# The first two query tiles of a fused attention and feed-forward kernel: another way to their scores and values, two more unsplit units, and a score block moved

## Chip, cores and metric

One core of one Trainium2 chip runs the whole program. The metric is the device time of that core in microseconds, the median of several executions. Five engines matter: TensorE (PE in the profile; PEld is its weight load), VectorE (DVE), ScalarE (ACT), GpSimd (POOL) and SyncE (SP), which issues all transfers.

## What is computed

Attention of 12288 queries over 768 pooled keys, and then two feed-forward layers. All widths are 128 (C), the hidden width F is 2048.

```python
kv_pool = kv.reshape(B, H // r, r, W // r, r, C).mean(axis=(2, 4))     # r = 4: 16 pixels a key
kv_flat = kv_pool.reshape(B, -1, C) @ w_sr                             # 768 x 128
k = v = kv_flat
s = scale * (q @ k.transpose(0, 2, 1))                                 # scale = 1/sqrt(128)
s = s - s.max(-1, keepdims=True)
a = np.exp(s); a /= a.sum(-1, keepdims=True) + 1e-09
x = a @ v
h = x @ w_in1;  g = where(h >= 1, h, where(h <= -1, 0, (h + 1)**2 / 4));  y1 = g @ w_out1
h = y1 @ w_in2; g = h * sigmoid(1.702 * h);                               out = g @ w_out2
```

## The kernel before

**Layout.** Everything lies with channels, keys or hidden columns on the 128 partitions and queries along the free axis. The queries come in 24 tiles of T = 512. A tile needs scores in KC = 6 chunks of 128 keys, a maximum over keys, the exponential, values (six chunks again), a division by the sum, and U = 8 *units* for each layer. A unit is 256 hidden columns: `layer_in` makes 128 x 1024 hidden values in PSUM, ScalarE and VectorE apply the nonlinearity, and `layer_out` adds the unit's part into `ps_y1` or `ps_y2`.

**Split arithmetic.** Precision comes from splitting each operand into an upper (fp32r) and a lower part and running three one-pass matmuls (`three_passes`, L469 to L471: upper by upper, upper by lower, lower by upper). The lower parts of the hidden values are made by GpSimd (`lower`, L380), the upper ones by VectorE (L1043) for layer 1. A *plain* unit does without: `layer_out_plain` (L595) multiplies unsplit fp32 values by the raw weights, as two matmuls, each of them two records in the trace. In the kernel before, the first PLAIN = U = 8 units of layer 1, the whole of tile 0, are plain in their output half.

**Pools and first keys.** Twelve groups of 64 keys arrive by 512 KB transfers (L311). VectorE sums each (`TENSOR_REDUCE`, L882) into `window_sum`. TensorE runs 16 records of matmuls whose result nobody reads while the sums arrive (L704), then projects keys (L476) and values (L482). Keys and the first queries are split, and tiles 0 and 1 are scored in three passes a chunk.

**Tile 0** has its own path. VectorE takes the maxima from PSUM, folds them to 32 rows, and spreads them with an identity pattern into `spread_hi` and `spread_lo`, which twelve matmuls with `minus_ones` subtract in PSUM (L523). ScalarE takes exponentials out of PSUM (L767). Values are six plain matmuls `v_sb` by `s_sb` (L554), with channels on the partitions. In parallel VectorE adds the keys (`add_first_keys`), matmuls sum over partitions (L532), VectorE inverts, a matmul spreads the inverse (L538), ScalarE copies it, and VectorE multiplies into `x_hi`, `x_sb` and `x_lo` (`normalise_first`).

**Later tiles.** The scores are copied to SBUF (by ScalarE for tiles 1 to 3, `evacuate`), VectorE folds the maxima (`maximum`, `fold_maximum`), SP stores the 512 maxima to DRAM and loads them back over all partitions (`spread_max`), VectorE subtracts (`shift`, L993), ScalarE exponentiates (L773), VectorE adds over keys (`add_keys`, L999) and inverts (`invert`, which holds the small `TENSOR_TENSOR` of L1015), and SP spreads the inverse in the same way. `normalise` and `x_lower` follow.

**Order.** Each engine has its list written by hand. From iteration 4 on it is a loop body: the scores of tile `it`, the values of tile `it-2`, then eight steps k. Step (it, k) runs layer 1's unit n = 8*it + k - 18 and layer 2's unit n = 8*it + k - 29, with the output halves two and one steps behind. The three iterations before this are written out: steps (2, 2) to (2, 7), then the values of tile 1 and the scores of tiles 2 and 3 together, then steps (3, 0) to (3, 7). GpSimd has its own list, in which the splits of the weights `w_in1`, `w_in2`, `w_out2` and `w_out1` (numbers 0, 2, 3, 1) lie between the waits, and `w_out1`'s lower halves are made in place of the raw weights only after the plain units have used them.

## Time and profile before

| | us |
|---|---|
| median of 3 runs (1302.08 to 1303.64) | 1302.35 |
| profiled execution, its own time | 1302.89 |
| its span in the trace | 1301.1 |
| PE busy | 1272.7 (98%) |
| POOL busy | 1140.8 (88%) |
| ACT busy, DVE busy | 1006.5, 1002.9 (77% each) |

The profiled time is 1.8 us more than the span. Most of the span is the loop, in which each of the 24 tiles takes the same time; the first tenth holds the hand-written start. A row of the timeline gives start, duration, engine, line, operation, output and inputs, the number of instructions merged, and in brackets the idle time before them and what ended it. The records of neighbouring matmuls overlap, so the pitch from one start to the next is what a matmul costs.

### The profile page before, as it was taken

What the parts mean: (1) busy time and instruction counts of PE and PEld (TensorE: products, weight loads), DVE (VectorE), ACT (ScalarE), POOL (GpSimd) and SP (SyncE); (2) the same over time, 40 slices, a digit from 0 to 9 for tenths busy, and PEclk for the clock granted to TensorE, in tenths of its full rate; (3) what the DMA queues carried; (4) which work ended last, traced back from release to release, by engine and by line L of the source; (5) the groups of instructions that cost most, each with busy time, mean ns of one, the idle gap of its engine ahead of it and who ended that gap; (6) DMA issues with size and microseconds to landing.
All of it is one profiled execution on the core that took longest, in us unless ns stands there. A gap on an engine that the chain in (4) does not pass through costs nothing.

```text
span 1301.1 us, 17012 instructions
## 1 busy us (share of the span) xinstructions
PE 1272.7 (98%) x5492; PEld 1027.3 (79%) x5492; DVE 1002.9 (77%) x1151; ACT 1006.5 (77%) x1069; POOL 1140.8 (88%) x476
## 2 busy tenths in 40 slices
PE   6989999999999999999999999999999999999998
PEld 4456888888888888888888888888888888888876
DVE  7877878779778787797797877967978878776443
ACT  3677787888877878888778788878787888797666
POOL 3538999999999999999999999999999999979780
PEclk9999999999999999999999999999999999999999
DMA  9010001000000010010000000100001000000000
GB/s 345 28 33 9 17 17 33 17 18 33 16 16 16 16 32 16 16 32 16 16 16 16 32 16 16 32 16 16 16 16 32 16 17 25 9 17 17 1 9 17
DMA packets 18258, 35.72 MB, mean 27 GB/s; under 512 B 3248, under 2 KB 3376, under 8 KB 17968
## 3 DMA queue, kind: packets, MB, share of 16 engines
q1 hardware_dynamic: 18224, 35.30, 8.3%
q8 instruction: 18, 0.29, 0.1%
q14 instruction: 16, 0.13, 0.0%
HBM read 28.90 MB, written 6.39 MB: 27 GB/s over the span
## 4 chain that ended last, share of the span: by engine, by line
PE 89%; POOL 5%; issue 3%; DVE 1%; ACT 1%; DMA 1%; POOLq 0%; SPq 0%; ACTq 0%; DVEq 0%
PE ps_ring L469 17%; PE ps_ring L471 16%; PE ps_ring L470 16%; PE ps_y L469 13%; PE ps_y L470 12%; PE ps_y L471 12%; POOL g_lo L380 4%; PE ps_y L595 1%; PE ps_y L554 1%; DMA kv_sb<-in_kv_t 1%; PE ps_k L704 0%; POOL pt_lo L380 0%; DVE g L1052 0%; POOLq L48 0%; DVE s_third L993 0%
## 5 line engine op out<-in xcount | busy, mean ns | idle before, releaser
L380 POOL TENSOR_TENSOR g_lo<-g,g_hi 128x1024 fp32r<-128x1024 f32 x365 | 930.2, 2577 | 89.7 <-DVE g L1052 80.0
L1043 DVE SCALAR_TENSOR_TENSOR g_hi<-g,ps_ring 128x1024 fp32r<-128x1024 f32 x184 | 223.9, 1217 | 145.0 <-ACT g L815 142.9
L796 ACT ACTIVATE g<-ps_ring 128x1024 f32<-128x1024 f32 x192 | 197.2, 1027 | 171.5 <-PE ps_ring L471 171.3
L469 PE MATMUL ps_y<-g_hi,w_hi 128*128 128x512 f32 x752 | 296.7, 394 | 8.1 <-POOL g_lo L380 6.9
L470 PE MATMUL ps_y<-g_lo,w_hi 128*128 128x512 f32 x752 | 293.2, 390 | 0.0
L471 PE MATMUL ps_y<-g_hi,w_lo 128*128 128x512 f32 x752 | 293.0, 390 | 0.0
L1052 DVE SCALAR_TENSOR_TENSOR g<-g,ps_ring 128x1024 f32<-128x1024 f32 x192 | 232.9, 1213 | 5.0 <-ACT g L815 5.0
L815 ACT ACTIVATE g<-g 128x1024 f32<-128x1024 f32 x192 | 204.3, 1064 | 5.4
L808 ACT ACTIVATE g<-ps_ring 128x1024 f32<-128x1024 f32 x192 | 197.7, 1030 | 8.6 <-PE ps_y L595 6.4
L798 ACT ACTIVATE g_hi<-ps_ring 128x1024 fp32r<-128x1024 f32 x192 | 195.8, 1020 | 6.2 <-PE ps_y L471 6.2
L469 PEld LDWEIGHTS ps_y<-g_hi,w_hi 128*128 128x128 f32 x752 | 141.1, 188 | 46.8 <-POOL g_lo L380 10.6
L471 PEld LDWEIGHTS ps_y<-g_hi,w_lo 128*128 128x128 f32 x752 | 141.3, 188 | 29.9
L470 PEld LDWEIGHTS ps_y<-g_lo,w_hi 128*128 128x128 f32 x752 | 141.4, 188 | 28.1
L469 PE MATMUL ps_ring<-x_hi,w_hi 128*128 128x512 f32 x382 | 151.7, 397 | 0.7 <-ACT s_sb L733 0.7
L380 POOL TENSOR_TENSOR pt_lo<-s_sb,pt_hi 128x1024 fp32r<-128x1024 f32 x60 | 151.4, 2552 | 0.0
L469 PE MATMUL ps_ring<-y_hi,w_hi 128*128 128x512 f32 x384 | 150.1, 391 | 0.0
L470 PE MATMUL ps_ring<-y_lo,w_hi 128*128 128x512 f32 x384 | 149.9, 390 | 0.0
L471 PE MATMUL ps_ring<-y_hi,w_lo 128*128 128x512 f32 x384 | 149.6, 390 | 0.0
L471 PE MATMUL ps_ring<-x_hi,w_lo 128*128 128x512 f32 x382 | 148.7, 389 | 0.0
L470 PE MATMUL ps_ring<-x_lo,w_hi 128*128 128x512 f32 x382 | 148.7, 389 | 0.0
L993 DVE TENSOR_TENSOR s_sb<-s_sb,key_max 128x1024 f32<-128x1024 f32 x66 | 126.5, 1919 | 0.0
L896 DVE COPY s_sb<-ps_ring 128x512 f32<-128x512 f32 x120 | 80.9, 688 | 52.7 <-PE ps_ring L471 52.7
(127 smaller groups left out, 1680.4 us busy)
## 6 DMA issues: line engine op xcount, KB each, us to landing
kv_sb<-in_kv_t SPq DMA_DIRECT2D x12, 512.0 KB, 9.0
q_sb<-in_q_t SPq DMA_DIRECT2D x24, 256.0 KB, 3.7
out_t<-y_sb SPq DMA_DIRECT2D x24, 256.0 KB, 3.6
key_max<-max_row SPq DMA_DIRECT2D x23, 256.0 KB, 3.4
inv_sum<-inv_row SPq DMA_DIRECT2D x23, 256.0 KB, 3.3
w_raw<-in_moe_w_in SPq DMA_DIRECT2D x2, 1024.0 KB, 17.4
max_row<-max_turned SPq DMA_DIRECT2D x23, 2.0 KB, 1.3
inv_row<-inv_turned SPq DMA_DIRECT2D x23, 2.0 KB, 1.3
```

What stands on the lines that cost most here:

```text
L380: return nc.gpsimd.tensor_tensor(dst, src, upper.bitcast(F32), ALU.subtract)
L469: nc.tensor.matmul(dst, l_hi, r_hi, start=start, stop=False)
L470: nc.tensor.matmul(dst, l_hi, r_lo, start=False, stop=False)
L471: return nc.tensor.matmul(dst, l_lo, r_hi, start=False, stop=stop)
L796: nc.scalar.activation(g2[:, slot, :], ps_h2(it, k), ACT.Gelu_apprx_sigmoid).then_inc(g2_done, 1)
L798: nc.scalar.activation(g2_hi[:, slot, :], ps_h2(it, k), ACT.Gelu_apprx_sigmoid).then_inc(g2_hi_done, 1)
L808: nc.scalar.activation(g, ps_h1(it, k), ACT.Relu, bias=0.5, scale=0.5).then_inc(relu_done, 1)
L815: nc.scalar.activation(g, g, ACT.Square).then_inc(square_done, 1)
L896: nc.vector.tensor_copy(s_sb[:, half, c, :], ps_s(it, c)).then_inc(s_evac, 1)
L993: nc.vector.tensor_tensor(pair, pair, key_max[:, :].unsqueeze(1).to_broadcast([P, 2, T]), ALU.subtract).then_inc(shifted, 1)
L1043: nc.vector.scalar_tensor_tensor(out=g1_hi[:, uu % 2, :], in0=g1[:, uu % 2, :], scalar=1.0, in1=ps_h1(it, k), op0=ALU.min, op1=ALU.max).th ...
L1052: nc.vector.scalar_tensor_tensor(out=g, in0=g, scalar=1.0, in1=ps_h1(it, k), op0=ALU.min, op1=ALU.max).then_inc(g1_done, 1)
```

## The change

1. **Tile 0 and 1 are scored by projected queries.** `w_sr` is transposed by a matmul, the queries are projected by it (`project_q`), and the score chunk is one plain matmul of `window_sum` by the projected queries (`whole_scores`). It needs neither projected keys nor split queries. The 16 unread matmuls are gone.
2. **GpSimd sums four of the twelve groups** (0, 3, 6, 9) by a tree of four additions; VectorE sums eight and takes the maxima of the score chunks between them.
3. **One spread of the maxima** with upper and lower part on different partitions: six matmuls in place of twelve.
4. **Tile 0's values with queries on the partitions**: for each key chunk four plain matmuls with 128 queries as weights and 129 moving columns, the last of them ones, so that the sums stand beside the values. ScalarE copies them out, and four matmuls by a diagonal of the inverses turn and scale them (`first_inputs`).
5. **Tile 1's score chunks 1 to 5 move** to after tile 0's values, between the first steps of layer 1.
6. **PLAIN = U + 2**: units 0 and 1 of tile 1 are plain too. `w_out1`'s lower parts are made in three pieces: units 2 and 3, units 4 to 7, and units 0 and 1 late.
7. **Tile 3 is scored after steps (3, 0) and (3, 1)**, not together with tile 2. ScalarE's, VectorE's and GpSimd's lists follow.

```diff
-        PLAIN = U
+        PLAIN = U + 2
+            def wait_sums(eng, group):
+                by_pool = sum(1 for g in POOL_GROUPS if g <= group)
+                at_least(eng, summed, group + 1 - by_pool)
+                at_least(eng, pool_summed, by_pool)
...
# GpSimd
+            def sum_windows(turn, g):
+                keys = slice(g * GK, (g + 1) * GK)
+                pool.wait_ge(kv_loaded[g], 16)
+                for level, width in enumerate((8, 4, 2)):
+                    if level:
+                        pool.wait_ge(windows_halved, turn * 3 + level)
+                    nc.gpsimd.tensor_tensor(kv_sb[:, keys, 0:width], kv_sb[:, keys, 0:width],
+                                            kv_sb[:, keys, width:2 * width], ALU.add).then_inc(windows_halved, 1)
+                pool.wait_ge(windows_halved, turn * 3 + 3)
+                nc.gpsimd.tensor_tensor(window_sum[:, keys].unsqueeze(2), kv_sb[:, keys, 0:1], kv_sb[:, keys, 1:2],
+                                        ALU.add).then_inc(pool_summed, 1)
...
-            q_lower(0, q_lo[:, :], q_sb[:, 0, :], q_hi[:, :])
-            pool.wait_ge(k_copied, 1)
-            pool.wait_ge(k_hi_done, 1)
...
+            for turn, g in enumerate(POOL_GROUPS):
+                sum_windows(turn, g)
             w_upper(0, 0)
+            pool.wait_ge(max_masked, 1)
             w_lower(0, 0)
-            pool.wait_ge(max_masked, 2)
             w_upper(0, 1)
             w_lower(0, 1)
-            pool.wait_ge(x_lo_done, 1)
+            pool.wait_ge(k_copied, 2)
+            pool.wait_ge(k_hi_done, 2)
+            pool.wait_ge(inverse_masked, 1)
+            lower(k_lo[:, :], k_sb[:, :], k_hi[:, :]).then_inc(k_lo_done, 1)
...
-            pool.wait_ge(g1_used, PLAIN - U // 2)
-            w_lower(1, 0)
+            pool.wait_ge(g1_used, U // 2)
+            w_out1_lower(PLAIN - U, U // 2 - 1)
+            pool.wait_ge(g1_used, U)
+            w_out1_lower(U // 2, U - 1)
             for k in range(U):
                 step(3, k)
-                if k == 4:
+                if k == 6:
                     pool.wait_ge(g1_used, PLAIN)
-                    w_lower(1, 1)
+                    w_out1_lower(0, PLAIN - U - 1)
...
# TensorE
+            def whole_scores(t, c):
+                if c == 0:
+                    pe.wait_ge(q_copied, t + 1)
+                if t == 0:
+                    wait_sums(pe, 2 * c + 1)
+                nc.tensor.matmul(ps_s(t, c), window_sum[:, c * P:(c + 1) * P], q_proj[:, t, :], start=True,
+                                 stop=True).then_inc(scores_ready, 1)
...
+                for b in range(QUADS):
+                    last = nc.tensor.matmul(ps_o_turned(b), s_sb[:, 0, c, b * P:(b + 1) * P], v_sb[:, c, 0:C + 1],
+                                            start=(c == 0 and b % 2 == 0), stop=(c == KC - 1), skip_group_check=True)
...
+                for b in range(QUADS):
+                    last = nc.tensor.matmul(ps_y1[:, b * P:(b + 1) * P], o_t[:, b, :], inv_diag[:, b, :], start=True,
+                                            stop=True)
...
+            turn_projection()
+            project_q(0)
+            for c in range(FIRST_CHUNKS):
+                whole_scores(0, c)
+            project_v(0)
             project_k(0)
...
+            whole_scores(0, 4)
+            project_q(1)
+            whole_scores(0, 5)
+            whole_scores(1, 0)
+            project_v(1)
+            project_k(1)
+            subtract_maximum()
             for c in range(KC):
-                score_chunk(1, c)
...
-            sum_first_keys()
-            value_chunk(0, 4)
-            spread_inverse()
-            value_chunk(0, 5)
-            for k in range(U):
+                first_values(c)
+            whole_scores(1, 1)
+            first_inputs()
+            whole_scores(1, 2)
+            step(2, 0, 2)
+            whole_scores(1, 3)
+            whole_scores(1, 4)
+            pe.wait_ge(s_early, 3)
+            step(2, 0, 3)
+            whole_scores(1, 5)
+            pe.wait_ge(s_early, 5)
+            for k in range(4, U):
                 step(2, 0, k)
-            values_then_scores(1, 2, 3)
-            for k in range(U):
+            values_then_scores(1, 2)
+            for k in range(2):
+                step(3, 1, k)
+            for c in range(KC):
+                score_chunk(3, c)
+            step(3, 1, 2)
+            pe.wait_ge(s_early, 3 * KC)
+            for k in range(3, U):
                 step(3, 1, k)
             iterations(pe, iteration)
...
# ScalarE, from the first step on
             step(2, 0, 2)
+            evacuate_chunk(1, 1, 3)
+            evacuate_chunk(1, 1, 4)
             step(2, 0, 3)
+            evacuate_chunk(1, 1, 5)
             step(2, 0, 4)
+            step(2, 0, 5)
             exponential(1, 1, 0)
-            step(2, 0, 5)
             exponential(1, 1, 1)
+            step(2, 0, 6)
             exponential(1, 1, 2)
-            step(2, 0, 6)
             step(2, 0, 7)
             evacuate(2, 0)
-            evacuate(3, 1)
+            step(3, 1, 0)
+            step(3, 1, 1)
+            for c in range(4):
+                evacuate_chunk(3, 1, c)
             x_upper(1, 1)
-            for k in range(U):
+            evacuate_chunk(3, 1, 4)
+            evacuate_chunk(3, 1, 5)
+            for k in range(2, U):
                 step(3, 1, k)
...
# VectorE, after tile 0
             maximum(1, 1, 2)
-            normalise_first()
             fold_maximum(1)
-            unit_full(2, 2)
-            unit_full(2, 3)
+            unit_full(2, 4)
+            unit_full(2, 5)
             shift(1, 1, 0)
-            unit_full(2, 4)
             shift(1, 1, 1)
             shift(1, 1, 2)
-            unit_full(2, 5)
+            unit_full(2, 6)
+            unit_full(2, 7)
             for p in range(PAIRS):
                 add_keys(1, 1, p)
-            unit_full(2, 6)
             invert(1)
-            unit_full(2, 7)
             for p in range(PAIRS):
                 maximum(2, 0, p)
             fold_maximum(2)
+            unit_full(3, 0)
+            unit_full(3, 1)
             normalise(1)
             x_lower(1, 1)
-            for p in range(PAIRS):
-                maximum(3, 1, p)
+            maximum(3, 1, 0)
+            shift(2, 0, 0)
+            maximum(3, 1, 1)
+            shift(2, 0, 1)
+            maximum(3, 1, 2)
...
-                if k < U - 1:
+                if 1 < k < U - 1:
                     unit_full(3, k)
...
                 if k == 2:
                     shift(2, 0, 2)
+                if k == 3:
+                    fold_maximum(3)
```

## Rows read from the trace of the kernel before

**Rows 1.** Busy time by stretch: us, then busy us and instructions of each engine

```profile
88.10:123.00 34.90, 28.62 (x105) 20.47 (x105) 30.70 (x33) 26.48 (x27) 27.74 (x12) 0.95 0.08 23
135.00:1301.10 1166.10, 1160.54 (x5093) 952.98 (x5091) 898.70 (x1017) 925.55 (x973) 1066.91 (x431) 1.00 0.06 19
```

**Rows 2.** The key groups' transfers: issues (ns, first to last start), and time to landing

```profile
L311 SPq DMA_DIRECT2D kv_sb<-in_kv_t x12: 417/442/655, 1.2 to 7.6; - x12
...
DMA to landing us min/median/max: 3.9/9.0/12.9
```

**Rows 3.** Timeline of tile 0: DVE, ACT, PE, and ACT at the first unit

```profile
9.01 12.71 DVE L882 TENSOR_REDUCE window_sum<-kv_sb 128x64 f32<-128x1024 f32 x10 [1.49 <-DMA kv_sb<-in_kv_t]
...
31.73 2.85 ACT L767 ACTIVATE s_sb<-ps_ring 128x1024 f32<-128x1024 f32 x3 [1.22 <-PE ps_ring L523]
...
32.90 3.67 PE L554 MATMUL ps_y<-s_sb,v_sb 128*128 128x512 f32 x8 [0.30 <-ACT s_sb L767]
...
43.74 1.03 ACT L808 ACTIVATE g<-ps_ring 128x1024 f32<-128x1024 f32 x1 [1.92 <-PE ps_ring L589]
```

**Rows 4.** Timeline of plain matmuls before 19 us: PE, then its weight loads

```profile
11.63 2.47 PE L704 MATMUL ps_k<-window_sum,w_k 128*128 128x256 f32 x5 [11.63 <-DVE window_sum L882]
...
17.62 0.86 PEld L482 LDWEIGHTS ps_v<-w_v,window_sum 128*128 128x128 f32 x7 [0.24 <-issue]
```

**Rows 5.** Groups by form, 0 to 60 us: GpSimd's subtractions (busy us, mean ns)

```profile
L380 POOL TENSOR_TENSOR w_lo<-w_raw,w_hi 128x1024 fp32r<-128x1024 f32 x5 | 11.9, 2385 | 0.2
...
L380 POOL TENSOR_TENSOR k_lo<-k_sb,k_hi 128x256 fp32r<-128x256 f32 x2 | 1.4, 730 | 9.8 <-ACT k_sb L733 9.8
```

**Rows 6.** Timeline of PE: plain output halves of two steps that follow each other

```profile
50.44 1.88 PE L595 MATMUL ps_y<-g,w_raw 128*128 128x512 f32 x4
...
53.54 1.88 PE L595 MATMUL ps_y<-g,w_raw 128*128 128x512 f32 x4
```

**Rows 7.** Timeline of ACT: tile 2's score chunks copied out

```profile
66.14 1.30 ACT L733 ACTIVATE s_third<-ps_ring 128x512 f32<-128x512 f32 x2 [0.38 <-PE ps_ring L471]
```

**Rows 8.** Groups by form, 40 to 110 us, DVE

```profile
L1052 DVE SCALAR_TENSOR_TENSOR g<-g,ps_ring 128x1024 f32<-128x1024 f32 x12 | 14.5, 1206 | 5.0 <-ACT g L815 5.0
...
L993 DVE TENSOR_TENSOR s_third<-s_third,key_max 128x1024 f32<-128x1024 f32 x3 | 3.6, 1214 | 0.0
```

**Rows 9.** Timeline of DVE: tile 2's last maximum and the end of its fold

```profile
69.13 1.25 DVE L919 TRANSPOSE_TENSOR_REDUCE part_max<-s_third 128x32 f32<-128x1024 f32 x1 [0.41 <-ACT s_third L733]
...
71.63 0.20 DVE L936 STREAM_TRANSPOSE max_turned<-row_max 32x32 f32<-32x32 f32 x1
```

**Rows 10.** The page's DMA issues: count, KB each, us to landing

```profile
key_max<-max_row SPq DMA_DIRECT2D x23, 256.0 KB, 3.4
...
max_row<-max_turned SPq DMA_DIRECT2D x23, 2.0 KB, 1.3
```

**Rows 11.** Timeline of POOL and DVE where both read SBUF

```profile
46.23 4.71 POOL L380 TENSOR_TENSOR w_lo<-w_raw,w_hi 128x1024 fp32r<-128x1024 f32 x2
...
49.55 2.48 DVE L993 TENSOR_TENSOR s_sb<-s_sb,key_max 128x1024 f32<-128x1024 f32 x1
...
102.20 7.13 POOL L380 TENSOR_TENSOR g_lo<-g,g_hi 128x1024 fp32r<-128x1024 f32 x3
...
107.44 2.97 DVE L993 TENSOR_TENSOR s_sb<-s_sb,key_max 128x1024 f32<-128x1024 f32 x1
```

**Rows 12.** PE's longest idle time after the first unit, and a stretch behind it

```profile
92.64 0.47 PE L469 MATMUL ps_y<-g_hi,w_hi 128*128 128x512 f32 x1 [4.38 <-POOL g_lo L380]
...
94.00:95.00 1.00, 1.00 (x4) 0.81 (x3) 0.00 (x0) 0.98 (x2) 1.00 (x1) 0.50 0.02 8
```

**Rows 13.** Timeline of ACT, DVE and PE at the junction with the loop

```profile
97.25 1.03 ACT L796 ACTIVATE g<-ps_ring 128x1024 f32<-128x1024 f32 x1 [1.24 <-PE ps_ring L471]
...
110.33 1.21 DVE L1043 SCALAR_TENSOR_TENSOR g_hi<-g,ps_ring 128x1024 fp32r<-128x1024 f32 x1
...
132.98 0.50 PE L469 MATMUL ps_y<-g_hi,w_hi 128*128 128x512 f32 x1 [0.59 <-POOL g_lo L380]
```

More of the change, by code:

```diff
@@ L394, in w_lower, with w_out1_lower @@
                 lower(w_lo[:, cols], w_raw[:, cols], w_hi[:, cols]).then_inc(w_lo_done[m], 1)
+            def w_out1_lower(first, last):
+                cols = slice(WF + first * 2 * P, WF + (last + 1) * 2 * P)
+                pool.wait_ge(w_hi_done[1], WP)
+                lower(w_lo[:, cols], w_raw[:, cols], w_hi[:, cols]).then_inc(w_lo_done[1], 1)
             def step(it, k):
@@ L510, in score_chunk @@
                 upper, lower = q_hi, q_lo
-                if is_number(t, 1):
-                    upper, lower = q1_hi, q1_lo
                 if is_number(t, 2):
@@ L518, in subtract_maximum @@
             def subtract_maximum():
-                pe.wait_ge(ones_ready, 2)
-                for part, spread in enumerate((spread_hi, spread_lo)):
-                    pe.wait_ge(max_masked, part + 1)
-                    for c in range(KC):
-                        last = nc.tensor.matmul(ps_s(0, c), minus_ones[:, :], spread[:, :], start=False,
-                                                stop=(part == 1), skip_group_check=True)
-                        if part == 1 and c % 2 == 1:
-                            last.then_inc(max_subtracted, 1)
@@ L528, in sum_first_keys @@
-            def sum_first_keys():
-                pe.wait_ge(s_early, KC)
-                pe.wait_ge(keys_added, 5)
-                for j in range(QUADS):
-                    last = nc.tensor.matmul(ps_y2[:, j:j + 1], key_sums[:, 4, j * P:(j + 1) * P], ones[:, 0:1],
-                                            start=True, stop=True)
-                last.then_inc(first_summed, 1)
-            def spread_inverse():
+                pe.wait_ge(ones_ready, 1)
+                pe.wait_ge(max_masked, 1)
@@ L537, in spread_inverse, with first_inputs @@
+            def first_inputs():
+                pe.wait_ge(o_copied, 2)
                 pe.wait_ge(inverse_masked, 1)
-                nc.tensor.matmul(ps_y2[:, :], ones[:, :], key_sums[:, 0, :], start=True,
-                                 stop=True).then_inc(sums_spread, 1)
+                for b in range(QUADS):
+                    last = nc.tensor.matmul(ps_y1[:, b * P:(b + 1) * P], o_t[:, b, :], inv_diag[:, b, :], start=True,
+                                            stop=True)
+                last.then_inc(x_turned, 1)
@@ L553, in value_chunk @@
                         pe.wait_ge(exp_done, t * PAIRS + (c // 2 + 1))
-                    nc.tensor.matmul(ps_o(t), v_sb[:, c, :], s_keys(t, t % 2, c), start=(c == 0),
+                    nc.tensor.matmul(ps_o(t), v_sb[:, c, 0:C], s_keys(t, t % 2, c), start=(c == 0),
                                      stop=(c == KC - 1)).then_inc(pv_done, 1)
@@ L799, in step @@
                                          ACT.Gelu_apprx_sigmoid).then_inc(g2_hi_done, 1)
+                if k == 3 and is_iteration(it, 3):
+                    y1_upper(it, 1 - half)
                 exists, tt, uu, n = unit(it, k, FIRST1)
@@ L808, in step @@
                     nc.scalar.activation(g, ps_h1(it, k), ACT.Relu, bias=0.5, scale=0.5).then_inc(relu_done, 1)
-                if k == 3 and is_tile(it - 3):
-                    act.wait_ge(g1_used, (it - 3) * U + U)
-                    at_least(act, h2_ready, (it - 4) * U)
-                    copy(y1_hi[:, 1 - half, :], ps_y1[:, :]).then_inc(y1_hi_done, 1)
+                if k == 3 and is_tile(it - 3) and not is_iteration(it, 3):
+                    y1_upper(it, 1 - half)
                 if exists:
```

352 lines of the change are left out of this document (182 added, 170 removed).

## The prediction, made before the changed kernel was run

> **What bounds the kernel now.** I read the engines' busy time by stretch first, and the reader should see in it where time can be won at all. From 135 us on TensorE is busy for 1160.5 of 1166.1 us, while no other engine is [rows 1]. The change leaves that part alone, so all it can do is to let this saturated part begin earlier or later. Between 88 and 123 us TensorE is busy for 28.6 of 34.9 us only [rows 1]: there other engines set the pace. The question is therefore by how much the junction moves at which TensorE waits for the last time, 132.98 us [rows 13]. Then I read the timelines of all engines from 0 to 135 us and followed back what released what. The order of each engine is written by hand, so I lay the changed lists out against each other with durations from this trace. Times below are positions from the span's start.
>
> **Tile 0, first part.** The last kv transfer is issued at 7.6 and lands 12.9 later, at 20.5 [rows 2]. VectorE's ten sums from 9.01 take 1.27 each and so end at 21.7 [rows 3]. Four sums moved to GpSimd do not bring this forward, because the transfer sets it; they free VectorE for maxima. GpSimd's tree adds 512, 256, 128 and 64 elements. Subtractions of 1024 and 256 elements took 2.385 and 0.730 [rows 5], so 2.16 ns an element and 0.18 fixed: 960 elements and four instructions give 2.8, with waits between them 3.2. The short strided runs have no row: the lower bound is 2.8, the upper 4.8, double fixed and element cost for the three small levels. I take 3.2. Groups land about 1.27 apart, so group 9 is there at 17.9 and summed at 21.1, just behind VectorE's pace. Score chunk 4, the projection of tile 1's queries and chunk 5 follow, plain matmuls of 512 columns. A plain one costs 0.86, half of the 1.73 for two that is worked out below from [rows 6]. That gives 23.7. Maximum 0.7, fold and spread 2.3, six subtracting matmuls, of which the first pair is out after 0.7: exponentials from 27.55, against 31.73 [rows 3]. The gain is 4.2.
>
> **Tile 0, second part.** Values start 1.17 behind the first exponential [rows 3], at 28.7. They are 24 matmuls of two records. Seven weight loads of such 128-column records took 0.86 with the last one's 0.19 in it, so 0.11 a record and 0.22 a matmul [rows 4]; sum 5.3, end 34.0. In the old form six chunks at 0.86 make 5.2, so nothing is won there; what goes is the four waits for sums, inverse, its spread and its copy. Small VectorE work on the sums and the diagonal takes 1.2, four turning matmuls 0.9 plus a start, splitting 0.7, the first unit 1.4: its result is out at 38.6. ScalarE took it at 43.74 before [rows 3]. The gain stands at 5.1.
>
> **Tile 1, where it is given back.** Three whole score chunks behind the first unit cost 3 x 0.86 = 2.6 of TensorE, and ScalarE has four more copies to do between the first activations. The unit pace was one step in 3.10 [rows 6]; now activation, square and VectorE's 1.2 [rows 8] of unit 0 and 1 wait behind those copies. VectorE reaches tile 1's last maximum at 46.0 and ends its fold at 48.4 (maximum 1.25 and fold 1.45 after it [rows 9], less overlap). Maxima go through DRAM: 1.3 and 3.4 [rows 10], so the first shift is at 53.1. Then, in ScalarE's new order, two exponentials of tile 1 stand ahead of unit 4: shift 1.2, shift 1.2, exponential 1.0, unit 4's two activations 2.0, exponential 1.0, unit 5's 2.0. That ends at 61.5. TensorE's values of tile 1 end at 61.2 and tile 2's scores follow at ScalarE's pace, 1.30 for two copies after 0.38 of waiting [rows 7], so 5.5 for six chunks with the start: 66.7. Two steps of 3.1 bring TensorE to 73.0. VectorE meanwhile does unit 5, three key sums, the inversion 2.5, three maxima, the fold and unit 6: 61.5 + 1.2 + 3.5 + 2.5 + 3.5 + 1.4 + 1.2, so 74.7 with the gaps. Tile 3's scores wait for this (1.5 idle). x_lo of tile 1 is ready 4.7 later at 79.3, and two steps and a unit (3.1 + 3.1 + 1.4) put the end of unit 10's input at 86.9. In the old trace that point is 92.64 - 4.38 = 88.3 [rows 12]. Of 5.1 won, 1.4 is left.
>
> **The wait behind it.** Before, TensorE idles 4.38 for GpSimd's split of the first split unit, and the following matmuls run at granted clock 0.50, 1.2 GHz [rows 12]. Now units 8 and 9 are plain. Each costs more: a plain step is 3.10, of which six input passes at 0.227 are 1.36, so its output half takes 1.73 against 1.36 split, twice 0.37. What TensorE waits for next is y1's lower part (same bank `ps_y1`). Here a lock decides. A shift that alone takes 1.21 [rows 8] took 2.48 at 49.55, and the subtraction on GpSimd ended at 50.94, 1.39 later; at 107.44 it took 2.97, with GpSimd busy until 109.33 [rows 11]. So VectorE's two-input subtraction in SBUF waits until GpSimd's running instruction ends. In the new lists `w_out1`'s four-unit piece starts on GpSimd when plain unit 7 is done, 6.25 after x_lo, and takes 2.4; tile 2's last shift asks 6.9 after x_lo. It loses 1.75 and ends at 89.0; y1_lo follows at 89.7. Plain unit 8 ends at 91.4, its follower's activations at 93.5, then a table load 1.3, and the first layer 2 activation starts at 94.8, against 97.25 [rows 13]: gain 2.4.
>
> **To the junction.** Units 10 and 11 pass ScalarE and VectorE at the same pace as before, so VectorE ends tile 2's sums with the 2.4. Behind them the old trace lost 1.9 to the lock (107.44 + 2.97 against 1.21). In my layout GpSimd has two fewer hidden subtractions behind it, its subtraction ends at 105.9 and unit 12 comes at 107.0, against 110.33 [rows 13], gain 3.3; if the small addition of 1e-9 in `invert` just misses a gap on GpSimd, all comes 0.9 later, gain 2.4. From there the pattern repeats the old one, since the last `w_out1` piece (1.3) fits into GpSimd's room. VectorE copies tile 4's scores, TensorE waits on them as before, and the junction moves by the same 2.4 to 3.3. I take 2.8.
>
> **The sum.** Span 1301.1 - 2.8 = 1298.3; with the 1.8 outside it, 1300.1 against the profiled 1302.89. That execution lies 0.5 above the median 1302.35, so I forecast 1302.35 - 2.8 = 1299.6.
>
> **Rivals.** (A) *Gains end in slack, no change.* GpSimd's trees at their upper bound delay chunk 4 by 1.6, another loss of the lock costs 0.9 to 1.8, and each moves the chain whole; together the gain is between 2.6 and none: 1299.8 to 1302.4, say 1301.0. For it: the chain has six hand-overs, each placed to a few tenths. (B) *The cold array, slower.* Without the 16 unread records TensorE does little before 20 us. In rows 4 five records of 256 columns in two passes took 2.47, so 0.43 a record, while the later records of 128 columns took 0.11, a quarter for half the columns: the array ran at 1.2 GHz first and at 2.4 GHz later. If it is still at 1.2 GHz until the values are through, chunk 4, the projection, chunk 5 (2.6) and the values (5.3) double: 7.9 against 2.8 won, 1307.4. It decides from 2.8 us of full-speed matmul work on the path that runs at the low clock: chunk 4, the projection and chunk 5 alone (2.6) just take the gain away. Against it: with chunks that cost 1.7 at 1.2 GHz, TensorE is nearly always busy from about 13 us on, as it was before from 11.63, and there the records at 17.62 were the short ones [rows 4]. (C) *More gain.* The last shift of tile 2 gets in ahead of GpSimd (0.65 decides), 1.75 more: 1297.8. (D) *The clock falls again.* TensorE idles 2.8 ahead of plain unit 8, where 4.38 was followed by the low clock [rows 12]; plain unit 8 then costs 1.7 more: 1301.3, within A's time.
>
> The Trainium skill, in "TensorE: Matmul & The Clock Gate", section "Part 1: The HAM clock gate", says that the throttled clock is the default state and activity releases it; that speaks for B, and no row shows how much activity the new start would need.
>
> **Chances.** My forecast with C: 0.50 (C 0.12 of it). A with D: 0.40. B 0.10. A measurement of this kernel tells about 0.2%, 2.6 us, from no change, and the forecast of 2.8 sits on that border, so faster by more is 0.50, within 0.2% is 0.41, and slower by more, B's upper half, is 0.09. The likeliest case's own range is 1297.8 to 1300.7. The whole range leaves out B and the best end of C: 1297.0 to 1303.0.
>
> **What the new profile would show.** First activation of a unit near 38.7 on ScalarE; exponentials of tile 0 near 27.6; weight loads of the turned values 0.11 apart; plain unit 8 near 89.7 behind y_lo; no stretch at clock 0.50 around 94; first layer 2 activation near 94.8; TensorE's last wait near 130.2. I am wrong if the first TensorE records near 20 are still 0.85 apart, if GpSimd's sum of group 9 ends after 22, or if the distance between old and new already differs by more than a microsecond at unit 10's input (86.9 against 88.3).

## The result, and the profile after

The changed kernel takes 1305.7 us (median of 11 runs, 1302.98 to 1308.87). The kernel before, run beside it, takes 1302.95 (11 runs, 1302.08 to 1303.83). The ratio is 1.0022 with a 95% interval from 1.0013 to 1.003, so the change costs 2.75 us and does not win the forecast 2.8. The time lies outside the predicted range, on the other side. The profiled execution took 1305.87, its span is 1304.1. Of the runs of the kernel before that stand beside the experiments, one took 4013.32 us and enters no number below.

The busy times of the changed kernel's page (first part), and the two stretches that answer to [rows 1]:

```profile
PE 1275.8 (98%) x5494; PEld 1023.8 (79%) x5494; DVE 989.8 (76%) x1138; ACT 1006.3 (77%) x1070; POOL 1143.8 (88%) x491
```

```profile
88.10:123.00 34.90, 30.27 (x103) 19.15 (x101) 30.51 (x35) 28.14 (x29) 20.36 (x9) 0.95 0.07 23
135.00:1304.10 1169.10, 1163.06 (x5107) 955.41 (x5105) 901.50 (x1020) 928.45 (x977) 1069.94 (x432) 1.00 0.06 19
```

The loop is as saturated as before. All that the change does happens ahead of the junction, and the junction came later. Its wait, to be set beside the last line of [rows 13], in the timeline of TensorE:

```profile
137.01 0.50 PE L502 MATMUL ps_y<-g_hi,w_hi 128*128 128x512 f32 x1 [0.55 <-POOL g_lo L408]
```

That is 4.03 later than before, while the span is only 3.0 longer: the loop gives 1.0 back, of which more below. The same points that the prediction gave, as it had them, before, and after:

| point | predicted | before | after | after less predicted |
|---|---|---|---|---|
| exponentials of tile 0 start (ACT) | 27.55 | 31.73 | 30.49 | 2.9 |
| first activation of unit 0 (ACT) | 38.6 | 43.74 | 42.21 | 3.6 |
| tile 1's folded maximum stored (SP) | 48.4 | 44.27 | 51.69 | 3.3 |
| first shift of tile 1 (DVE) | 53.1 | 49.55 | 57.46 | 4.4 |
| unit 8's input starts (PE) | 79.3 | 80.10 | 84.50 | 5.2 |
| plain unit 8 (before: split unit 8) | 89.7 | 92.64 | 95.20 | 5.5 |
| first activation of layer 2 (ACT) | 94.8 | 97.25 | 102.17 | 7.4 |
| upper part of unit 12 (DVE) | 107.0 | 110.33 | 114.36 | 7.4 |
| junction (PE) | 130.2 | 132.98 | 137.01 | 6.8 |

The error is made in three places: 2.9 ahead of the exponentials, 2.3 between there and unit 8's input, 1.9 between plain unit 8 and layer 2. The first place, in the timeline of TensorE:

```profile
9.99 2.07 PE L524 MATMUL ps_ring<-q_proj,window_sum 128*128 128x512 f32 x2 [0.69 <-ACT q_proj L801]
...
13.20 3.58 PE L524 MATMUL ps_ring<-q_proj,window_sum 128*128 128x512 f32 x4 [1.13 <-POOL window_sum L404]
...
18.69 1.15 PE L524 MATMUL ps_ring<-q_proj,window_sum 128*128 128x512 f32 x2 [1.91 <-DVE window_sum L977]
19.65 1.89 PE L532 MATMUL ps_two<-wsr_sb,window_sum 128*128 128x128 f32 x8
21.34 1.89 PE L538 MATMUL ps_two<-window_sum,wsr_sb 128*128 128x512 f32 x2
23.05 1.04 PE L524 MATMUL ps_ring<-q_proj,window_sum 128*128 128x512 f32 x2
```

and the same microseconds as stretches (the last three columns are the granted clock, the share of the DMA engines, and GB/s):

```profile
20.00:21.00 1.00, 1.00 (x7) 1.00 (x6) 1.00 (x2) 0.00 (x0) 0.66 (x2) 0.50 1.06 438
21.00:22.00 1.00, 1.00 (x4) 0.67 (x4) 1.00 (x2) 0.42 (x1) 0.00 (x0) 0.50 1.00 418
22.00:23.00 1.00, 1.00 (x2) 0.33 (x1) 0.82 (x1) 0.18 (x1) 0.00 (x0) 0.50 0.95 322
```

There are two slow times here. The first chunk takes 2.07, twice the 1.02 to 1.04 of the same two records later, so TensorE starts at 1.2 GHz; within chunks 1 and 2 it gets faster, and chunk 3 costs 0.96 from its start to the next, at 2.4 GHz. Ahead of chunk 3 TensorE had waited 1.91 for a sum; behind chunk 3 the granted clock falls to 0.50, 1.2 GHz, for some 3.5 us. The two projections of keys and values take 1.89 each, and chunk 4 starts at 23.05 and not at 21.1. GpSimd is not the cause; its last tree, group 9, is through at 20.74:

```profile
17.84 2.53 POOL L401 TENSOR_TENSOR kv_sb<-kv_sb 128x512 f32<-128x512 f32 x3 [0.94 <-DMA kv_sb<-in_kv_t]
20.45 0.29 POOL L404 TENSOR_TENSOR window_sum<-kv_sb 128x64 f32<-128x64 f32 x1
```

Behind the exponentials the price list holds. 48 records of the turned values take 5.60 (predicted 5.3), ScalarE has the first unit's result 11.7 after its first exponential (predicted 11.1):

```profile
31.66 5.60 PE L587 MATMUL ps_two<-v_sb,s_sb 128*128 128x129 f32 x48 [0.27 <-ACT s_sb L850]
```

```profile
30.49 2.86 ACT L850 ACTIVATE s_sb<-ps_ring 128x1024 f32<-128x1024 f32 x3 [1.16 <-PE ps_ring L572]
...
42.21 1.02 ACT L898 ACTIVATE g<-ps_ring 128x1024 f32<-128x1024 f32 x1 [1.04 <-PE ps_ring L647]
```

The maxima of tile 1 then go through DRAM. The second of these issues waits until the first has landed, so their distance is the first's time: 2.31, where it was 1.34 before. Timelines of the DMA queue's issues and of VectorE:

```profile
51.69 0.34 SPq L343 DMA_DIRECT2D max_row<-max_turned  x1
54.00 0.34 SPq L346 DMA_DIRECT2D key_max<-max_row  x1
```

```profile
57.46 1.23 DVE L1060 TENSOR_TENSOR s_sb<-s_sb,key_max 128x1024 f32<-128x1024 f32 x1 [1.66 <-DMA key_max<-max_row]
```

The third place is the wait ahead of plain unit 8. VectorE's last shift of tile 2 waits for GpSimd's piece of `w_out1`, as forecast, and `y_lo` stands behind it. VectorE, GpSimd and TensorE, in three timelines, and the clock of the stretch:

```profile
91.27 3.27 DVE L1060 TENSOR_TENSOR s_third<-s_third,key_max 128x1024 f32<-128x1024 f32 x1
94.47 0.68 DVE L968 TENSOR_TENSOR y_lo<-ps_y,y_hi 128x512 fp32r<-128x512 f32 x1
```

```profile
91.08 2.38 POOL L408 TENSOR_TENSOR w_lo<-w_raw,w_hi 128x1024 fp32r<-128x1024 f32 x1 [16.92 <-PE ps_y L653]
```

```profile
95.20 3.44 PE L653 MATMUL ps_y<-g,w_raw 128*128 128x512 f32 x4 [2.81 <-DVE y_lo L968]
```

```profile
96.00:97.00 1.00, 1.00 (x2) 0.34 (x1) 0.90 (x5) 0.48 (x1) 0.00 (x0) 0.50 0.00 0
```

The shift takes 3.27 for the 1.21 of [rows 8]; it ends 1.08 after the subtraction whose end it waited for, as in [rows 11]. The idle time is 2.81 (forecast 2.8), and what I had put at the end of the list of rivals follows: the clock falls, and four records take 3.44 in place of 1.88 [rows 6].

### The profile page after: what moved, and what is told of

It reads as the page before. It is cut to its first block, busy times and chain, and to the rows that moved or that the text cites. A ratio compares the mean times of both kernels' runs of the same rounds, so it can differ in the third digit from the quotient of the medians.

```text
span 1304.1 us, 17033 instructions
## 1 busy us (share of the span) xinstructions
PE 1275.8 (98%) x5494; PEld 1023.8 (79%) x5494; DVE 989.8 (76%) x1138; ACT 1006.3 (77%) x1070; POOL 1143.8 (88%) x491
## 3 DMA queue, kind: packets, MB, share of 16 engines
HBM read 28.90 MB, written 6.39 MB: 27 GB/s over the span
## 4 chain that ended last, share of the span: by engine, by line
PE 87%; POOL 5%; issue 3%; DVE 2%; ACT 1%; DMA 1%; POOLq 0%; SPq 0%; ACTq 0%; DVEq 0%
PE ps_ring L502 16%; PE ps_ring L503 16%; PE ps_ring L504 16%; PE ps_y L502 12%; PE ps_y L503 12%; PE ps_y L504 12%; POOL g_lo L408 4%; DMA kv_sb<-in_kv_t 1%; PE ps_y L653 1%; PE ps_ring L524 0%; PE ps_two L587 0%; DVE s_third L1060 0%; POOL pt_lo L408 0%; DVE part_max L1000 0%; ACT g L898 0%
```

## The experiments

Three questions: is the low clock at 20 us and at 96 us the cause of the loss; what else lies on the path; and which parts of the change pay. The kernels were timed in three groups (e1 to e4, e5 to e8, e9 to e12), each group on one chip beside the kernel before (medians 1302.89, 1302.91 and 1303.19). None leaves out any of the computation. The stations are the exponentials of tile 0, the first shift of tile 1, the junction, and the first store of maxima in the loop (before 143.73, after 147.75).

| kernel | median us | ratio to before (95%) | exponentials | shift | junction | store in the loop |
|---|---|---|---|---|---|---|
| before | 1302.95 | | 31.73 | 49.55 | 132.98 | 143.73 |
| after | 1305.70 | 1.0022 (1.0013 to 1.003) | 30.49 | 57.46 | 137.01 | 147.75 |
| e1_unread | 1304.21 | 1.0009 (1.0 to 1.0018) | 28.24 | 55.58 | 135.21 | 145.98 |
| e2_y1_first | 1304.89 | 1.0013 (1.0004 to 1.0022) | 30.26 | 57.16 | 134.34 | 145.14 |
| e3_both | 1301.97 | 0.9994 (0.9985 to 1.0003) | 28.14 | 55.40 | 132.57 | 143.34 |
| e4_old_no_unread | 1303.74 | 1.0006 (0.9996 to 1.0015) | 32.80 | 50.63 | 134.60 | 145.39 |
| e5_load_first | 1301.43 | 0.9987 (0.9978 to 0.9996) | 28.25 | 55.03 | 132.20 | 142.96 |
| e6_plain8 | 1304.33 | 1.0011 (1.0002 to 1.002) | 28.23 | 55.60 | 135.08 | 145.85 |
| e7_sums_dve | 1301.33 | 0.9987 (0.9978 to 0.9996) | 28.90 | 55.00 | 132.16 | 142.91 |
| e8_unit4_first | 1303.55 | 1.0003 (0.9994 to 1.0012) | 28.14 | 56.45 | 134.29 | 145.06 |
| e9_fill | 1306.02 | 1.0026 (1.0015 to 1.0037) | 30.29 | 57.51 | 135.64 | 146.41 |
| e10_fill_unread | 1303.43 | 1.0005 (0.9996 to 1.0014) | 28.37 | 55.85 | 134.64 | 145.38 |
| e11_three | 1301.18 | 0.9991 (0.9982 to 1.0) | 29.27 | 55.26 | 132.39 | 143.14 |
| e12_plain12 | 1303.48 | 1.0004 (0.9995 to 1.0013) | 29.35 | 55.25 | 133.27 | 145.24 |

### e1: unread matmuls in the new start

```diff
+            def unread(cols):
+                nc.tensor.matmul(ps_s(0, KC - 1)[:, 0:cols], wsr_t[:, :], q_sb[:, 0, 0:cols], start=True, stop=True)
             for c in range(FIRST_CHUNKS):
                 whole_scores(0, c)
+                if c == 0:
+                    unread(256)
+                if c == 2:
+                    unread(512)
```

> The changed kernel with two unread matmuls put back into TensorE's idle time before chunk 3 (256 and 512 columns). Theory 1 (TensorE at 1.2 GHz from 19.5 to 23 us is what delays the start): those records run at 2.4 GHz, chunk 5 ends near 24.3 in place of 26.3, tile 0's exponentials start near 28.5 in place of 30.5, and the time falls by 2 us to about 1303.7, with less scatter from run to run. Rival (the start is delayed by the hand-overs between engines, and the clock only fills waits): less than 0.5 us.

Two matmuls are added, and the junction comes 1.8 earlier. TensorE's timeline, to be read beside the first fence of after above: chunk 3 starts 0.59 earlier, and the two projections take 1.05 and 1.02 in place of 1.89 each. The 0.59 comes by way of VectorE, which takes the maximum of chunk 2 ahead of the sum that chunk 3 waits for: it starts on it at 16.23, and at 16.82 in the changed kernel, where TensorE's chunks before it were slower.

```profile
18.10 1.13 PE L524 MATMUL ps_ring<-q_proj,window_sum 128*128 128x512 f32 x2 [1.05 <-DVE window_sum L984]
19.07 1.05 PE L532 MATMUL ps_two<-wsr_sb,window_sum 128*128 128x128 f32 x8
19.96 1.02 PE L538 MATMUL ps_two<-window_sum,wsr_sb 128*128 128x512 f32 x2
20.92 1.10 PE L524 MATMUL ps_ring<-q_proj,window_sum 128*128 128x512 f32 x2
```

The exponentials move by 2.25, the shift by 1.88, the junction by 1.80; the median by 1.5, and the runs draw together (1302.77 to 1304.66). The low clock of the start, early and behind chunk 3 together, is worth this much. The second low stretch is still there, behind an idle time of 2.82, and the kernel is still slower than before: the start alone does not explain the loss.

### e2 and e3: `y1_lo` ahead of tile 2's last shift

```diff
                 if k == 3:
...
                     lower(y1_lo[:, 0, :], ps_y1[:, :], y1_hi[:, 0, :]).then_inc(y1_lo_done, 1)
+                    shift(2, 0, 2)
                 unit_upper(3, k)
                 if 1 < k < U - 1:
                     unit_full(3, k)
-                if k == 2:
-                    shift(2, 0, 2)
```

> The changed kernel with VectorE's y1_lo ahead of tile 2's last shift. Theory 1 (that shift waits 2.1 us for GpSimd, TensorE idles 2.8 us behind it and then runs at 1.2 GHz for three more): TensorE's idle time ahead of plain unit 8 falls below 0.6 us, no stretch at clock 0.50 follows, and layer 2's first activation comes 4 us earlier, at 98; the time falls by 3 to 4 us, to about 1302.2. Rival (the shift, not y1_lo, is what the chain needs: the exponentials of tile 2 and unit 10's activation stand behind it): the idle time goes, but the activation comes less than 1.5 us earlier and the time falls by less than 1.5.

> Both edits. Theory 1: the gains add, 5 to 6 us below the changed kernel, about 1300, which is 2 to 3 us below the kernel before and what was forecast. Rival: within 1 us of the better of the two.

In e2 TensorE goes on to plain unit 8 at once, at full clock, and waits 1.43 one step later:

```profile
92.10 1.98 PE L653 MATMUL ps_y<-g,w_raw 128*128 128x512 f32 x4
95.51 0.47 PE L502 MATMUL ps_ring<-y_hi,w_hi 128*128 128x512 f32 x1 [1.43 <-DVE g L1119]
```

The junction comes 2.67 earlier; the median only 0.8, below what I expected. The runs scatter from 1302.78 to 1305.73; why the median does not follow the trace is not shown. With both edits (e3) the junction comes 4.44 earlier, which is 1.80 and 2.67 together, and at 132.57 it is just ahead of the old one. The runs lie between 1301.51 and 1302.43. So the low clock of the start, and the wait with the low clock behind it, together account for 3.7 us of the median; what is left of the change gains 0.9 against the kernel before, within what can be told, and not the forecast 2.8.

### e4: the kernel before without its unread matmuls

```diff
-            for g in range(4, FIRST_GROUPS):
-                pe.wait_ge(summed, g)
-                for _ in range(2):
-                    nc.tensor.matmul(ps_k[:, 3, 0:4 * GK], w_k[:, :], window_sum[:, 0:4 * GK], start=True, stop=True)
```

> The kernel before without its 16 unread matmuls. Theory 1: its first records near 16.7 us run at 1.2 GHz and it loses 2 to 4 us, to about 1305.5, with more scatter. Rival (the old start has slack in its transfers and sums): under 0.7 us.

The exponentials come 1.07 later and the junction 1.62; the median is 0.8 above that of before, less than expected and not separable. The timeline shows where: the first projections run at the low clock, and the scores from the fourth record on do not.

```profile
16.26 2.04 PE L476 MATMUL ps_k<-window_sum,w_k 128*128 128x512 f32 x2 [16.26 <-DVE window_sum L878]
18.10 1.91 PE L482 MATMUL ps_v<-w_v,window_sum 128*128 128x128 f32 x8
20.38 0.77 PE L469 MATMUL ps_ring<-q_hi,k_hi 128*128 128x512 f32 x1 [0.37 <-POOL k_lo L380]
```

Before, the two took 1.04 and 1.05 from 16.74 on. In the traces the old start is therefore 1.62 better at the junction for its 16 matmuls; in the median the price is not shown.

### e5, e7, e11: the way of the maxima, and GpSimd's sums

Each is e3 with an edit. In e5 SP issues the load of tile 4's queries ahead of `spread_max(1)`:

```diff
             load_q(3)
-            spread_max(1)
             load_q(4)
+            spread_max(1)
```

> Both edits (the two unread matmuls, y1_lo first), and the load of query tile 4 issued ahead of the store of tile 1's maxima. Theory 1 (the 2 KB store takes 2.3 to 2.6 us in place of 1.3 because no transfer has run for 15 us or more): the store lands after 1.4 us, tile 1's first shift comes 1.1 us earlier than 55.40, and the junction with the loop moves with it, to 131.5. Rival (the store is slow for another reason, or the shift waits anyway): the shift stays within 0.3 us of 55.40.

The store still takes 2.38 (49.47 to 51.85), so the theory that an idle queue makes it slow has fallen. The median is 0.5 below that of e3, and the interval against the kernel before now leaves out 1.

In e7 VectorE makes all twelve sums again (groups 0 and 3 ahead of the first maximum):

```diff
-    POOL_GROUPS = (0, 3, 6, 9)
+    POOL_GROUPS = ()
...
             first_chunk_maximum(1)
-            first_chunk_maximum(2)
+            sum_windows(6)
             sum_windows(7)
+            first_chunk_maximum(2)
             sum_windows(8)
+            sum_windows(9)
             first_chunk_maximum(3)
```

> Both edits, with all twelve groups summed by VectorE. Theory 1 (the transfers set the sums' pace, and the maxima between them must fit beside): the last chunk's maximum comes after the sums and two maxima are pushed back, 1.0 to 1.5 us on tile 0's exponentials (28.14), same at the junction. Rival (GpSimd's tree of group 9 is the later one and VectorE alone is quicker): exponentials earlier than 28.1.

The exponentials start 0.76 later than in e3, and yet the first shift comes 0.40 earlier, because the store of the maxima takes 1.47 and not 2.60:

```profile
50.11 0.34 SPq L343 DMA_DIRECT2D max_row<-max_turned  x1
51.58 0.34 SPq L346 DMA_DIRECT2D key_max<-max_row  x1
```

So the lead that GpSimd's trees give is real, and in these two traces more than all of it is lost in the store; they bring the time nothing. What goes with a long store is shown in the last section; whether the trees would pay beside a short one was not tried. e11 has both edits, these two diffs on top of e3:

> The unread matmuls at the start, y1_lo first, tile 4's load first, all sums on VectorE. Theory 1 (each of the last two gave 0.4 us at the junction through the maxima's way over DRAM, by different parts of it): 142.5 for the loop's first store in place of 142.9, 1301.0 us. Rival (they give the same 0.4): 142.9, 1301.4.

Its median, 1301.18, is the lowest of the study, but not to be told from 1301.33 and 1301.43: the two gains do not add. The store takes 1.69 there. Any of the three can be kept: they lie 1.5 to 2.0 us below the kernel before by the medians, 1.2 to 1.7 by the ratios.

### e6 and e12: how many plain units

e6 is e3 with two plain units fewer and without the last `w_out1` piece, e12 is e11 with two more:

```diff
-        PLAIN = U + 2
+        PLAIN = U
...
-                if k == 6:
-                    pool.wait_ge(g1_used, PLAIN)
-                    w_out1_lower(0, PLAIN - U - 1)
...
```

```diff
-        PLAIN = U + 2
+        PLAIN = U + 4
...
-            pool.wait_ge(g1_used, U // 2)
-            w_out1_lower(PLAIN - U, U // 2 - 1)
...
-                if k == 6:
+                if k == 7:
                     pool.wait_ge(g1_used, PLAIN)
                     w_out1_lower(0, PLAIN - U - 1)
...
```

TensorE's waits for the pieces follow in both.

> Both edits, with units 0 and 1 of tile 1 split again (PLAIN = 8). Theory 1 (the two unsplit units pay by taking GpSimd's subtractions off the path, more than their 0.73 us on TensorE): TensorE waits for unit 8's lower part, 2 us or more, and the junction comes 1 to 3 us later than 132.57. Rival (with y1_lo early, GpSimd is no longer on the path there): within 0.7 us of 132.57.

> The same, with four unsplit units in tile 1 in place of two. Theory 1 (between 90 us and the junction the chain runs over VectorE and GpSimd, and each unsplit unit takes an upper part of 1.2 and a lower part of 2.4 off them for 0.37 on TensorE): the loop's first store 1 to 2.5 us earlier, near 141. Rival (the chain runs through tile 3's shifts, which the units do not touch, and the last piece of the weights now comes late): no gain, or a new wait at unit 16.

In e6 the old wait for GpSimd is back, with the low clock behind it:

```profile
95.07 0.77 PE L499 MATMUL ps_y<-g_hi,w_hi 128*128 128x512 f32 x1 [4.55 <-POOL g_lo L408]
```

The store in the loop is 2.5 later than in e3, and the median 2.4 higher. This part of the change is worth what the whole was forecast to win. In e12 the work up to 102 us is as in e11, and then TensorE waits 2.88 for a lower part at the junction, where e11 waits 0.58:

```profile
133.27 0.50 PE L500 MATMUL ps_y<-g_hi,w_hi 128*128 128x512 f32 x1 [2.88 <-POOL g_lo L408]
...
134.76 0.61 PE L500 MATMUL ps_ring<-y_hi,w_hi 128*128 128x512 f32 x1
135.17 0.63 PE L501 MATMUL ps_ring<-y_lo,w_hi 128*128 128x512 f32 x1
```

1.5 us after that wait the records go from 0.40 to 0.63 for three to four microseconds. The store in the loop comes 2.1 later than in e11. The median is 2.3 higher: two more plain units cost time.

### e8: unit 4 ahead of tile 1's exponentials

```diff
-            exponential(1, 1, 0)
-            exponential(1, 1, 1)
             step(2, 0, 6)
+            exponential(1, 1, 0)
+            exponential(1, 1, 1)
             exponential(1, 1, 2)
```

VectorE's list follows: `unit_full(2, 6)` ahead of the three shifts.

> Both edits, with unit 4 of tile 0 ahead of tile 1's shifts and exponentials on VectorE and ScalarE. Theory 1 (ScalarE idles for 4 us until the maxima are back while unit 4 lies ready, and then its 2.0 us stand in the chain): unit 5's square, tile 2's scores and all behind them come 1.0 to 2.0 us earlier, the junction near 131. Rival (the chain runs through tile 1's exponentials and values, not through the units): less than 0.4 us.

The store in the loop comes 1.7 later than in e3, against what I expected. TensorE now waits 2.73 for the exponentials, the clock falls, and the values of tile 1 take 7.09 in one go, where e3 needs 5.97 from start to end:

```profile
58.90 7.09 PE L612 MATMUL ps_y<-s_sb,v_sb 128*128 128x512 f32 x12 [2.73 <-ACT s_sb L863]
```

```profile
57.86 3.67 PE L612 MATMUL ps_y<-s_sb,v_sb 128*128 128x512 f32 x8 [1.66 <-ACT s_sb L863]
...
61.85 1.98 PE L612 MATMUL ps_y<-s_sb,v_sb 128*128 128x512 f32 x4 [0.32 <-ACT s_sb L863]
```

The first fence is e8, the second e3. The values start 1.04 later by the order and take 1.1 longer by the clock. In this trace the chain runs through tile 1's exponentials and values, and not, as I had thought, through the units. How much of the 1.7 is order and how much is clock, the trace does not separate; two runs of e8 without the low clock, given in the last section, speak for the clock.

### e9 and e10: the clock alone

To separate the clock from the wait, 11 unread one-pass matmuls fill the idle time ahead of plain unit 8 (e9 on the changed kernel; e10 has e1's two besides). The order of all other work stays.

```diff
+                    if is_number(n, U):
+                        pe.wait_ge(g1_done, U + 1)
+                        for _ in range(11):
+                            nc.tensor.matmul(ps_ring[:, 1, 0:T], w_hi[:, 0:P], x_hi[:, 1, :], start=True, stop=True)
```

> The changed kernel with eleven unread one-pass matmuls in the time in which TensorE waits for y1_lo ahead of plain unit 8. The wait itself stays. Theory 1 (the low clock behind the wait is a cost of its own, and idle time lets the clock fall): no stretch at 0.50 near 96, plain unit 8 starts within 0.3 us of 95.2 and layer 2's first activation comes 1.5 to 1.9 us earlier, near 100.5; the time falls by 1.5 us to 1304.2. Rival (the clock falls at a point of its own): the stretch at 0.50 stays and nothing moves by more than 0.5 us.

> The changed kernel with both kinds of unread matmuls (start, and ahead of plain unit 8) and no other edit: only TensorE's clock differs. Theory 1: the junction with the loop, 137.01 in the changed kernel, comes 1.8 + 1.6 earlier, at 133.6, and the time is about 1302.5, level with the kernel before: the clock is the whole of the measured loss. Rival (the clock costs less than the two windows suggest): above 1304.

In e9's trace the unit still waits for `y_lo` but runs at full clock:

```profile
92.31 2.67 PE L705 MATMUL ps_ring<-x_hi,w_hi 128*128 128x512 f32 x11
95.30 1.98 PE L653 MATMUL ps_y<-g,w_raw 128*128 128x512 f32 x4 [0.33 <-DVE y_lo L972]
```

Unit 8 takes 1.98 in place of 3.44, and the junction comes 1.37 earlier. The median does not follow: 1306.02 in 7 runs (1303.59 to 1307.02), while the profiled execution itself took 1304.52. So on e9's times alone the low clock behind the wait is not shown to cost anything. Five of the seven runs have a mean granted clock of 1.000, and so have six of the changed kernel's eleven: a stretch as long as the one at 96 us, 3.4 us at half clock, would make that 0.999, so in those runs of the changed kernel there was nothing at 96 us for the fill to mend. e10 came out 2.3 below the changed kernel, with its junction 2.37 earlier where 1.80 and 1.37 would make 3.17. In its trace a new low stretch, behind an idle time of 1.90 ahead of tile 1's values, stands where the missing part can have gone:

```profile
60.00:61.00 1.00, 1.00 (x2) 0.40 (x2) 0.00 (x0) 0.97 (x2) 1.00 (x2) 0.50 0.00 0
```

With unread matmuls alone, the ratio to the kernel before is 1.0005 (0.9996 to 1.0014), where it was 1.0022. The clock thus makes up most of the measured loss: 1.5 of the median by the start (e1), and 0.8 more in e10.

## Why the prediction was wrong

**What bounds the kernel** was right: the loop is saturated in both, and everything is decided by the junction. One thing was missed. The junction is 4.03 later and the span only 3.0, because a tile of the loop takes 51.88 on average where it took 51.94 (loop stores from 199.53 to 1029.65, before 195.52 to 1026.54, 16 periods each). Why is open.

**Tile 0, first part: the step that failed.** "Group 9 is summed at 21.1" was right (20.74), and the plain chunks' 0.86 too, but only at 2.4 GHz. The step assumed TensorE ready for chunk 4 when the sums are. It was not: it was at 1.2 GHz and had the projections of keys and values, 3.4 us long, still ahead of chunk 4, which started at 23.05. Of the 2.9 us that this part missed, e1 returns 2.25; the sign named for it, first records near 20 still 0.85 apart, came true. This was rival B in its cause, a low clock on the path, and in part in its mechanism. B had TensorE slow because it had done little, and that holds for the first chunks (2.07). But TensorE did reach 2.4 GHz (chunk 3), and then fell back behind an idle time, which no rival had at this place. B was set at 0.10 with "nearly always busy from about 13 us on" against it; in fact VectorE puts maxima between its sums and TensorE waits 1.91 for one of them. Its price was mis-sized as well, in the other direction: 7.9, the whole path up to the values, where the clock was back at 23 and the loss at the junction is 1.8. Alone, 1.8 would have left 1.0 of the forecast 2.8; it takes the next terms to make a loss of it.

In "TensorE: Matmul & The Clock Gate", section "Part 1: The HAM clock gate", the Trainium skill says that the throttled clock is the default and activity releases it. Here the trace agrees: the first two records of 512 columns take 2.07, and only behind chunks 1 and 2 do two such records cost 0.96.

**Tile 0, second part** was right in its prices: 5.60 for 5.3 in the values, 11.7 for 11.1 from the exponentials to the unit.

**Tile 1** was right in structure, including that the gain is given back here; 3.7 was to be given back between unit 0's activation and the end of unit 10's input, and 5.7 was (from 1.53 earlier to 4.13 later, 92.39 for 88.26). One term was mis-sized: the store of the maxima, 1.3 by the page's median [rows 10], took 2.31. Even with the clock restored and the order of `y1_lo` changed (e3), unit 8's input starts at 82.45 against 79.3; of these 3.15, 0.6 lie ahead of the exponentials, 1.3 are the store (2.60 for 1.3), and the rest is tenths in the hand-overs, for which no single step was isolated.

**The wait behind it**: the lock was read rightly. The shift took 3.27 where 2.96 was forecast (1.21 and the 1.75 lost), and TensorE idled 2.81 for 2.8. What was missing from the sum is what that idle time does to the clock. It stood in the text as rival D, 1.7 us, and was put inside the no-change case as though it excluded the others. e9 gives 1.37 of it back at the junction in the trace, and moving `y1_lo`, which removes wait and low clock, gives 2.67 (e2).

**To the junction** was right in its better case, 0.9 gained: layer 2's first activation is 4.92 later than before, unit 12's upper part and the junction 4.03. The small addition of `invert` takes 0.17 (at 110.92) where it took 1.00. The old loss to the lock is 1.76 by [rows 11] (2.97 for 1.21), not the 1.9 of the text, and 1.71 of it is there still (2.92 at 111.53).

**Rivals.** A (no change) did not happen: GpSimd's trees were not late (20.74) and no further loss to the lock was found, only the tenths in the hand-overs; D and B happened together, which the chances had not allowed for, since each rival was priced with the others absent. C was not seen. The two unsplit units were worth the 2.4 of e6; four sums on GpSimd, nothing (e7).

**The account** of the 6.8 us at the junction of the profiled execution: 1.8 the clock at the start (e1), 1.4 the clock behind the wait (e9, by its trace), 1.0 the store, and 2.6 that are left over and were not separated.

## What to carry to other kernels

Unread matmuls ahead of a start may look like waste, and they are worth pricing before they are removed: ask of every new idle time of TensorE whether the clock will fall behind it, and charge the following matmuls double. When several rivals share a cause, here the clock, price them together and give them one chance. Before a second engine is brought in to make something earlier, look at whether the next hand-over (here a 2 KB store) passes the lead on. And where a profiled execution and the other runs show different mean clocks, an account of the one is not yet an account of the median.

## What the runs showed of the hardware

**Idle times and the clock.** A low stretch followed idle times of 1.91 (at 18.69 after, and in e2 and e9 at the same place), 2.81 (after), 2.82 (e1), 2.73 (e8), 2.88 (e12) and 1.90 (e10), and lasted three to four microseconds each time; so it did behind 4.38 (before), and behind 4.55 nearly seven (e6). None followed 1.43 (e2), 1.66 (e3) and 1.76 (e1, at the place of e10's 1.90). In e12 the fall came only 1.5 us after work had resumed; in e1 it came while TensorE was still idle.

**It does not fall in every run.** Each run comes with its mean granted clock. e3, e5, e7 and e11, whose traces show no low stretch, have 1.000 in all their 44 runs, and theirs scatter by 0.9 to 2.2 us, against the 5.9 of the changed kernel. e8 has 0.999 in nine runs (1303.37 to 1304.27) and 1.000 in two: 1301.29 and 1301.69. So unit 4's place need not cost anything when the clock stays. The kernel before has 0.997 in 74 of the 94 runs beside the experiments, with medians of 1303.28, 1303.11 and 1303.27 in the three groups, and 0.999 in 20, with 1301.96, 1301.64 and 1301.96: 1.3 to 1.5 us of its own time go with how long the clock is low. Its profiled execution is one of 0.999, with 3.4 us low behind the wait; e6, with the same kind of wait, has 0.997 and 6.8 us low there. The Trainium skill, same page and section, says of a kernel's start that the count of slow matmuls varies from run to run; these rows show a variation too, and e8's lies past the start.

**The column is blind at the start.** In e4 it reads 1.00 from 16 to 20 us, while the projections take 2.04 and 1.91, twice their full-speed time. Up to the first change of clock the durations alone tell. A mean of 1.000 therefore does not exclude a low clock at the start, and the changed kernel has six such runs between 1302.98 and 1305.7. Their median is 1304.9, still 1.9 above the kernel before, though the low stretch at 96 us cannot be in them: for these runs the second half of the account above does not hold. That these began at 1.2 GHz and stayed there longer than in the profiled one would fit, also with the scatter of e2 and e9, which have the same start; no trace shows it, and it stays open.

**A store of 2 KB** took 1.34, 1.46, 1.47, 1.69 and 2.30 to 2.60 in the start of different kernels, without an idle queue being the reason (e5). The long ones are the nine kernels in which GpSimd makes sums, the short ones the two old kernels and e7, e11 and e12. The DMA view shows what else differs. Here is what moved in GB/s, in slices of 0.1 us, after (first line, from 50.49) and in e7 (second line, from 48.91), the store issued at 51.69 and at 50.11:

```profile
GB/s 0 0 0 0 0 0 0 0 0 0 0 0 0 0 0 0 0 0 0 0 11 91 0 0 0 1 0 0 0 0 0 0 0 0 0 0 0 0 0 0
...
GB/s 0 0 0 0 0 0 0 0 0 0 0 0 0 82 0 0 0 0 0 0 12 9 0 0 0 0 0 0 0 0 0 0 0 0 0 0 61 82 184 246
```

The store is the 12 and 9; the 82, in the first line within the 91, is one 8 KB transfer of a queue that the view calls `q14 instruction`. In all nine long stores it falls into the store or up to 0.4 us behind its beginning, and the store's last piece moves 0.4 to 0.7 us after its first; in the five short ones it lies 0.5 to 1.9 us ahead, and the store is moved within 0.2. So a transfer of instructions goes with the long store in fourteen traces of fourteen. That it is the cause was not tried, and the slower movement is only about half of the 1 us that the landing is late; the rest is open.
